# The hand-over from attention to the first layer: where GpSimd does its splits and sums among the last three pairs of heads

## What is computed

```python
q_rot, k_rot = (rotate(q), rotate(k))
scores = scale * np.matmul(q_rot, k_rot.transpose(0, 1, 3, 2))
scores = scores - np.max(scores, axis=-1, keepdims=True)
attn = np.exp(scores)
attn = attn / (np.sum(attn, axis=-1, keepdims=True) + 1e-09)
attn_out = np.matmul(attn, v)
x = np.ascontiguousarray(attn_out.transpose(0, 2, 1, 3)).reshape(B * S, H * D)
h = x @ w_in; r = np.maximum(h, 0.0); x = (s * (r * r) + b) @ w_out     # layer 1
h = x @ w2_in; out = (h * (1.0 / (1.0 + np.exp(-1.702 * h)))) @ w2_out  # layer 2
```

## Time and profile before

| | |
|---|---|
| median of 3 runs | 1085.67 us (1085.67 to 1087.19) |
| the profiled execution | 1085.56 us |
| its span in the trace | 1083.7 us |
| TensorE busy | 1046.9 us, 97% of the span |
| VectorE, ScalarE, GpSimd busy | 733.1, 634.0, 706.8 us |
| mean granted TensorE clock | 0.995 |
| last instruction of attention's PV on TensorE | 321.4 us from the span's start |

### The profile page before, as it was taken

How to read it: one execution, slowest core, us unless ns; L and a number is a source line. 1 busy time by engine, 2 the same in 40 slices (tenths; PEclk the granted TensorE clock), 3 DMA queues, 4 the chain that set the end, 5 groups by cost and what they waited for, 6 DMA issues and landing times.

```text
span 1083.7 us, 17067 instructions
## 1 busy us (share of the span) xinstructions
PE 1046.9 (97%) x6234; PEld 965.3 (89%) x6234; DVE 733.1 (68%) x874; ACT 634.0 (59%) x1124; POOL 706.8 (65%) x587
## 2 busy tenths in 40 slices
PE   4899999999978999999999999999999999999998
PEld 4899999999967999999999999999898888898987
DVE  6888888888857656766576654865567655854542
ACT  4887878787755445645555544754465445654442
POOL 6878787878679764676466665666656674565430
PEclk9999999999989999999999999999999999999999
DMA  4555455554113221222122212122221412142101
GB/s 112 128 149 152 110 148 142 153 128 124 42 49 98 88 68 59 78 60 78 60 63 73 79 59 78 59 73 64 75 62 54 141 59 78 59 136 59 59 21 58
DMA packets 100613, 93.03 MB, mean 86 GB/s; under 512 B 15652, under 2 KB 78644, under 8 KB 100532
## 3 DMA queue, kind: packets, MB, share of 16 engines
q1 hardware_dynamic: 99408, 90.94, 29.7%
q10 hardware_dynamic: 1124, 1.02, 0.3%
HBM read 69.44 MB, written 4.79 MB: 68 GB/s over the span
## 4 chain that ended last, share of the span: by engine, by line
PE 68%; POOL 1%; DVE 0%; issue 0%
PE psum L1106 37%; PE psum L1078 31%; POOL wout_lo L1033 0%; POOL win_lo L1023 0%; POOL wsum L1007 0%; POOL wsum L1009 0%; POOL wsum L1006 0%; POOL wsum L1011 0%; DVE x_sums L1135 0%; POOL xT L581 0%
## 5 line engine op out<-in xcount | busy, mean ns | idle before, releaser
L1023 POOL TENSOR_TENSOR win_lo<-win_raw,win_hi 128x768 fp32r<-128x768 f32 x48 | 101.0, 2104 | 249.0 <-ACT win_hi L1017 249.0
L1078 PE MATMUL psum<-xc_hi,win_hi 128*128 128x384 f32 x672 | 227.0, 338 | 7.7 <-POOL xc_lo L558 4.0
L1078 PE MATMUL psum<-xc_lo,win_hi 128*128 128x384 f32 x672 | 226.8, 338 | 0.0
L1078 PE MATMUL psum<-xc_hi,win_lo 128*128 128x384 f32 x672 | 226.3, 337 | 0.0
L1078 PEld LDWEIGHTS psum<-xc_hi,win_hi 128*128 128x128 f32 x672 | 127.0, 189 | 17.4 <-POOL xc_lo L558 4.4
L1078 PEld LDWEIGHTS psum<-xc_lo,win_hi 128*128 128x128 f32 x672 | 126.9, 189 | 8.2
L1033 POOL TENSOR_TENSOR wout_lo<-wout_raw,wout_hi 128x1024 fp32r<-128x1024 f32 x48 | 119.8, 2495 | 16.5 <-ACT wout_hi L1235 16.5
L1078 PEld LDWEIGHTS psum<-xc_hi,win_lo 128*128 128x128 f32 x672 | 126.9, 189 | 0.0
L762 ACT ACTIVATE E<-psum,negmax 128x576 f32<-128x576 f32 x128 | 94.7, 745 | 13.1 <-DVE negmax L861 13.0
L861 DVE TENSOR_REDUCE negmax<-psum 128x1 f32<-128x576 f32 x128 | 90.9, 751 | 14.2 <-PE psum L627 13.6
L1027 DVE TENSOR_TENSOR win_lo<-wsum,win_hi 128x1024 fp32r<-128x1024 f32 x47 | 96.6, 2056 | 4.3 <-ACT win_hi L1017 4.1
(11 more groups left out here) (154 smaller groups left out, 2849.2 us busy)
## 6 DMA issues: line engine op xcount, KB each, us to landing
wout_raw<-in_moe_w_out_dram SPq DMA_DIRECT2D x48, 512.0 KB, 3.6
win_raw<-in_moe_w_in_dram SPq DMA_DIRECT2D x48, 256.0 KB, 2.8
win_raw<-in_moe_w_in_dram SPq DMA_DIRECT2D x96, 128.0 KB, 2.8
Q<-QK SPq DMA_DIRECT2D x60, 144.0 KB, 2.8
QK<-QK SPq DMA_DIRECT2D x30, 288.0 KB, 3.4
vraw<-in_v_dram SPq DMA_DIRECT2D x32, 128.0 KB, 2.5
raw<-in_q_dram SPq DMA_DIRECT2D x30, 128.0 KB, 2.9
raw<-in_k_dram SPq DMA_DIRECT2D x30, 128.0 KB, 2.8
```

Of the source, the lines that this page charges most:

```text
L1023: pool.tensor_tensor(win_lo[m % 2][:, 0:3 * BLK], win_raw[m % 2][:, 0:3 * BLK], win_hi[m % 2][:, 0:3 * BLK].bitcast(F32), ALU.subtract).th ...
L1078: mm = pe.matmul(hps(n, k), w[n % 2][:, at:at + P], x[k][:, t, :], start=k in FRESH and t == 0 and i == 0, stop=t == HK - 1 and i == 2, sk ...
```

## The change

Four things are moved, and nothing is added to or taken from the computation.

- GpSimd, attention: `win_low(0)` goes from the end of step 14 to between V0 and V1 of pair 14. `first_x(0)` goes from the end of step 14 to between V0 and V1 of pair 15. `first_x(1)` goes from behind `finish` of pair 14 to ahead of it. `w_sum(1)` goes from the end of step 15 to the end of step 14. `finish` of pair 15 is no longer part of attention's order.
- GpSimd, window 0: after `win_low(1)` come `wout_low(0)`, then `finish` of pair 15, then `w_sum(2)`.
- ScalarE: the copy P1 (`first`) goes from behind x splits 4, 5 and 6 to directly behind `wsplit`, with the fetch of PV0 behind it.
- VectorE: `block_11` of window 0 (`first`) and the fetch of PV0 (`sum0`) go ahead of x splits 4, 5 and 6.

```diff
-    ACT_ORDER = order("exp12@0 hi01@-1 exp13@0 first@-2 evac1@-2 qk0@2 hi02@-1 qk1@2 hi03@-1 hiQ@-1 hiT@-1 icp@-1 "
-                      "hi10@-1 hi11@-1 hi12@-1 hi13@-1 xc02@-1 xc03@-1 wsplit@-1 xc04@-1 evac0@-1 xc05@-1 xc06@-1 exp00@1 exp01@1 exp02@1 exp03@1 expT@1 "
+    ACT_ORDER = order("exp12@0 hi01@-1 exp13@0 evac1@-2 qk0@2 hi02@-1 qk1@2 hi03@-1 hiQ@-1 hiT@-1 icp@-1 "
+                      "hi10@-1 hi11@-1 hi12@-1 hi13@-1 xc02@-1 xc03@-1 wsplit@-1 first@-1 evac0@-1 xc04@-1 xc05@-1 xc06@-1 exp00@1 exp01@1 exp02@1 exp03@1 expT@1 "
...
-    POOL_ORDER = order("rot1@3 eps@0 V0@0 V1@0 vlo0@0 vlo1@0 finish@-1 rot0@4")
+    POOL_ORDER = order("rot1@3 eps@0 V0@0 mid@0 V1@0 vlo0@0 vlo1@0 late@0 finish@-1 rot0@4")
...
+                def between_values(p, _, __):
+
+                    if p == NPAIR - 2:
+                        win_low(pool, 0)
+                    if p == NPAIR - 1:
+                        first_x(0)
+
+                def after_values(p, _, __):
+
+                    if p == NPAIR - 1:
+                        first_x(1)
+
+                def finish_pair(p, _, __):
+
+                    if p < NPAIR - 1:
+                        finish(pool, p)
...
                     if s == NPAIR - 2:
-                        win_low(pool, 0)
-                        first_x(0)
-                    if s == NPAIR - 1:
-                        first_x(1)
                         w_sum(pool, 1)
...
                 if n + 1 < WINDOWS:
                     win_low(pool, n + 1)
+                if n == 0:
+                    wout_low(pool, 0)
+                    finish(pool, NPAIR - 1)
...
                 if n + 2 < WINDOWS:
                     w_sum(pool, n + 2)
-                wout_low(pool, n)
+                if n > 0:
+                    wout_low(pool, n)
```

More of the change, by code:

```diff
@@ L517, in attention_sync, with finish @@
                 program(SP_FIRST, SP_ORDER, {"load": load_next, "loadv": load_next_v, "qcopy": q_copies, "kcopy": k_copy, "put": put_inv, "get": get_inv}, after)
+            def finish(pool, p):
+                b, t = p // KT * S, p % KT
+                pool.wait_ge(evac_done, 2 * p + 2)
+                pool.wait_ge(half_done, 2 * p + 2)
+                pool.tensor_tensor(osum[p % 2][:], osum[p % 2][:], O[p % 2][:], ALU.add).then_inc(sum_done, 1)
+                pool.wait_ge(sum_done, p + 1)
+                pool.wait_ge(inv_in[p % 2], 48 * (p // 2 + 1))
+                pool.tensor_tensor(xT[:, t, b:b + MAIN].rearrange("d (p j) -> d j p", j=NM),
+                                   osum[p % 2][:, 0:MAIN].rearrange("d (j p) -> d j p", j=NM),
+                                   inv_row[:, 0:MAIN].rearrange("d (j p) -> d j p", j=NM), ALU.mult)
+                pool.tensor_tensor(xT[:, t, b + MAIN:b + S], osum[p % 2][:, MAIN:S], inv_row[:, MAIN:S], ALU.mult).then_inc(x_done, 1)
             def attention_gpsimd(pool):
@@ L601, in after @@
                     if s == NPAIR - 2:
-                        win_low(pool, 0)
-                        first_x(0)
-                    if s == NPAIR - 1:
-                        first_x(1)
                         w_sum(pool, 1)
-                program(POOL_FIRST, POOL_ORDER, {"rot": rotate_one, "V": hi_V, "vlo": lo_V, "finish": finish, "eps": add_eps}, after)
+                program(POOL_FIRST, POOL_ORDER, {"rot": rotate_one, "V": hi_V, "vlo": lo_V, "finish": finish_pair, "eps": add_eps, "mid": between_values, "late": after_values}, after)
             def attention_tensor(pe):
```

15 lines of the change are left out of this document (2 added, 13 removed).

## The result

| | before | after |
|---|---|---|
| median of 10 runs each | 1087.01 us (1085.49 to 1088.36) | 1084.21 us (1082.42 to 1084.50) |
| the profiled execution | 1085.56 us | 1082.42 us |
| its span | 1083.7 us | 1080.6 us |
| last instruction of attention's PV, end | 321.67 us | 313.88 us |
| product 4 of window 1, start | 340.64 us | 337.33 us |

The ratio is 0.9973 with an interval of [0.9964, 0.9983]: 2.8 us faster. The forecast was 1079.5 us, and its range ended at 1082.5. So the direction came true and the size did not.

The account below looks back on a forecast made before the run. Bound: TensorE's waits and low clock between 300 and 340 us. PV1 ends 7.2 us earlier, new waits for P5 and U leave 6.1; 1085.56 becomes 1079.4, plus 0.1 for the median: 1079.5 us, range 1076.0 to 1082.5.

Parts of the forecast that it names:

- win_low(0) fits the gap: GpSimd, ahead of pair 14's second V: win_low(0), 4.17 us, moves into a 4.18 us gap and costs nothing.
- VectorE's wait for eps: Pair 15's eps stood behind first_x(0), VectorE waiting 1.8 us; the wait goes, gaining 1.3 us (0.33 to 1.8).
- What is late next: After PV1: weight load behind inv_row reads at 315.95 us, new 4 us wait for P5, then 1 to 3 for U.
- The 1.94 us of idle: TensorE, window 1: the chain over h_a, gate and copy stays, so 1.94 us of idle remains.
- GpSimd's part: Block starts at 299.8 us; finish(14), now last, takes 3.5 and ends at 314.1; xc_lo ready at 310.6 instead of 315.3.
- a meeting: GpSimd operation beside a VectorE one: 0.7 us more each time, counted for first x pair, w_sum(2) and finish(15).
- VectorE's part: block_11 waits for product 1 ahead of three x splits; the split TensorE asks for at 316.6 is ready near 314.3, cost nothing.
- The start of the sum: Profiled execution of the kernel before, 1085.56 us, with the median of the runs taken as 0.1 above it.
- rival D: Late hand-over: clock falls again during the wait for U, or the load needs 5.1 us; 1080.6 to 1082.6, chance 0.12.
- E: Waits only change place: load longer behind inv_row reads, P5 hold over 8 us, U near old time; 1084.5, chance 0.08.
- C: Full exclusion: each of five meetings costs GpSimd VectorE's whole operation (1.28 us), 2.9 us more; 1082.4, chance 0.06.
- F: Slower: TensorE's clock stays at 1.2 GHz from product 1 to window 1's second y_part; 1090.5 us, chance 0.05.

Follow-up runs that it names:

- e1: Changed kernel with pair 15's three inv_row reads put behind the first two weight loads on SyncE; 1079.37 us, ratio 0.9927 to the kernel before.
- e2: Changed kernel with the low parts of x blocks 4 to 6 of the first chunk replaced by zeros from memset; 1080.32 us, ratio 0.9938.
- e5: Changed kernel with ScalarE's and VectorE's orders put back as before, GpSimd's new orders kept; 1082.08 us, ratio 0.9956 to the kernel before.
- e8: Changed kernel with VectorE's order alone put back as before, ScalarE's new order kept; 1082.64 us, ratio 0.9962 to the kernel before.
- e3: Changed kernel with finish(14) put back ahead of first_x(1) on GpSimd; 1085.61 us, ratio 0.9988 to the kernel before.

## Why the prediction had the direction and not the size

**What held.** win_low(0) fits the gap: its two operations ran from 287.39, and pair 14's second V at 291.58 has no idle ahead of it. VectorE's wait for eps is gone, PV0 started at the forecast 306.1, and with no wait for xc_lo at all (0.7 forecast) PV1 ended at 313.88, 0.6 earlier than forecast. "What is late next" named the right three: the load goes out directly behind the reads, TensorE is held for P5 (7.18 us, though, for a forecast 3 to 4.5), then for U (1.90; forecast 1 to 3). The clock fell in the first hold. e1 shows that the queue is the cause, and e2 gives the chain's times from the reads on to 0.2 us. That its finish(14) ended at 314.23, as forecast, is in part luck: even there it took 4.4 us and not 3.5, and started 0.8 earlier than I had it. The 1.94 us of idle that I left standing in window 1 came to 0.23 (1.12 in e2); it lies ahead of the wait for U, so this cost the sum nothing.

**The step that failed** is in GpSimd's part: "That took 3.04 us; with some stretching by VectorE I give it 3.5." It took 7.03. The 3.04 is pair 13's, which met no operation of VectorE with two inputs in SBUF; pair 14's own finish had already taken 3.83 before (307.51 to 311.34). I counted the two splits at 308 and not the three behind them, and priced a meeting by the earlier trace rows, where the GpSimd operation had lost 0.7. That price is right for the two large operations: 2.16 for 1.42, and 1.91 for 1.30. The third lost 2.6, since it met three splits in a row. All of it went through the reads to the load, to P5 and to U: product 4 of window 1 at 337.33, 2.8 later than the forecast 334.5, and the profiled execution at 1082.42 instead of 1079.4.

**The step that made it so** is in VectorE's part: "I cost this at nothing." I looked only at whether TensorE would get the splits in time, which it did. I did not ask what three reads of SBUF in a row would hold up on GpSimd. e5 and e8 give 1.2 to 1.8 us for it.

**The start of the sum** was too low as well. I put the median 0.1 us above the profiled execution, from three runs. Over ten runs the kernel before has a median of 1087.01, which is 1.45 above its profiled 1085.56; the changed kernel's median lies 1.8 above its own. So of the 4.7 us between 1079.5 and 1084.21, 3.0 come from the stage (1082.42 for 1079.4), 1.3 from the kernel before's median (1087.01 for 1085.67), and some 0.3 to 0.4 are left. As a gain the forecast was 6.1 us; it came to 3.1 between the profiled executions and 2.8 between the medians.

**The second fall of the clock** I had put into rival D with a chance of 0.12. After the wait for U it came in the traces of e2, e3, e5 and e8, and cost 1.5 us in each; the changed kernel's trace has no such fall. The wait that I forecast for U was about as long as the 1.7 us that ended in a low clock before, so a fall was worth more than that chance.

**The rivals.** E had the mechanism that came: the load waits longer behind the inv_row reads. Its 1084.5 is also nearest to the median of 1084.21. But its other signs did not come (a hold of over 8 us, U near its old time, a gain of 2 at most); the time lies between it and the forecast's chain. And what I held against it, that no load took over 5.1 us, was beside the point: the load went out late, and landed some 4 us after it was issued. C, the full exclusion, gave 1082.4, which the profiled execution met, though not by C's own sum: the first x pair lost nothing on GpSimd (1.48 and 1.85), and the meetings were not equal. The Trainium skill, "SBUF — State Buffer", section "Who interferes with whom", has the loser blocked for the whole instruction. This case agrees for most meetings: a GpSimd operation lost 0.6 to 0.74 us to a split of 0.95, and VectorE's two splits took 4.43 together, so each waited out a GpSimd operation. For the small multiply, and for win_low(1) in e5 and e8, the block was longer than one instruction. In the rival I had taken 1.28 as the length of VectorE's operation, and that figure already held its own waiting; the row of the operation alone (0.96 at 320.88 in the trace before) was the one to use, and where the whole row of splits goes first, times their number. F did not come: the clock was back at 2.4 GHz by 330 us, after 5.4 us of work at 1.2 GHz.

## What to carry to other kernels

A step that is moved on one engine moves whatever waits for it on an in-order DMA queue: read the queue behind it, and put the loads that the path needs ahead of reads that nobody needs soon (e1: 4.8 us for the order of three reads). Before two-input SBUF operations of VectorE are put together, look at what GpSimd does at that time, and give its operation a bound at the price of the whole row of them, be it small (2.6 us lost in the changed kernel) or large (2.3 in e8). And when a wait is removed, count TensorE's idle time over the whole stretch: here it was 9.95 and 9.37 us.
